# The first dense product placed ahead of the last row's attention values, and three copies of constants moved from the third to the last group of the first expert

## The chip, the cores and the metric

One Trainium2 chip, one of its cores. The metric is the device time of one execution in microseconds (us). Engines are named as the profile names them: PE is TensorE (PEld is its weight load), DVE is VectorE, ACT is ScalarE, POOL is GpSimd, SP is SyncE, which here only issues DMAs (SPq is its queue).

## What is computed

The program runs three layers after each other, all in float32 (here cut to what matters):

```python
# attention, B=2 H=8 S=768 D=64: only keys in the query's hash bucket count
scores = np.where(q_bucket[..., :, None] == k_bucket[..., None, :], scale * q @ k.T, -1e9)
x = softmax(scores) @ v                      # -> [1536, 512]
# first mixture, dense: every expert computes every token
P = sinkhorn(x @ w_gate)                     # 8 rounds of row and column sums
x = sum(P[:, e:e+1] * (relu(x @ w1[e]) @ w2[e]) for e in range(8))
# second mixture, routed: each token goes to one expert, or to none
out = x;  out[chosen] += gate * (relu(x @ w1[e_idx]) @ w2[e_idx])
```

## The kernel before

Each engine has its own program, and they meet at semaphores. The core's work comes in three stages: attention up to about 249 us, the dense mixture (8 experts of about 106 us) up to about 1157 us, then the routed one.

**Attention.** There are 96 row tiles of 128 queries (16 heads of 6). For each, PE computes the scores, turns the probabilities (`turn`, L1596) and multiplies them by the values (`values`, 18 small matmuls on L1606, L1608 and L1610). ACT evicts the turned probabilities as a rounded float16 part, and DVE takes the rest as a second part, `probsT_lo` (L1096). `values` of a tile waits for that. The last tile's `values` stands alone behind the loop over pairs of heads. DVE then scales its result (`normalise_last`, up to L1127), which lets PE turn the second batch's x (`turn_x`, L1641).

**An expert of the dense mixture.** The first matrix product is a fast scheme of 7 products instead of 8. `expert` on PE runs 8 groups (g = 0 to 7). A group is seven calls of `group_product`, six matmuls of 128x384 each (L1699, L1701, L1702). The first four write four PSUM banks, and the other three add into them. Each product needs the parts of one block of x (`x7_hi` and `x7_lo`), which POOL, ACT and DVE make from `xf`: POOL sums and splits on L687 to L705, ACT rounds on L852, DVE takes the remainder on L1153. In the first expert `x_parts` waits for them. DVE combines the banks (L1254, L1262 to L1269) and splits the result for the second product (L1258, L1351). ACT copies one bank (L927, `x1s`). Then PE runs 12 row tiles (t = 0 to 11) of the second product, 24 matmuls of 128x512 each (L1673, L1676, L1677), alternating between two banks, so tile t waits until DVE has emptied tile t - 2.

**What the first expert does besides.** The 8 rounds of the gate are woven into its 12 row tiles. Behind tile t DVE copies the tile out (L1306) and does one round of the gate (L1225 to L1243), ending in `columns_in`. Behind tile t PE waits for `columns_in` to reach t, and sums over the partitions with a small matmul (L1795). At t = 1, 2, 4, 5, 7, 8 and 10 DVE also makes the low part of a block of the next expert's first weights (`w1_part`, L1197), for which ACT must have made the high part (L896) from `wf`. ACT waits for all four loads of `wf`. POOL sums blocks of it (L625 to L636), each behind one more round of the gate.

**SP's queue.** SP issues its DMAs in the order of its program. After the second weights of expert 0 it stands as follows: SP first waits for three signs of `blank_ready`, two of which come from DVE's copies in the diff. `rows` is the buffer in HBM in which the routed stage collects tokens. The loop then brings the next expert's weights into `wf`, whose buffer is free once DVE has made the last part of w2 (behind group 6).

```python
sp.wait_ge(blank_ready, 3)
sp.dma_start(row_tiles, blank[...].to_broadcast(...)).then_inc(blanked, 16)   # L462
with sp.Fori(1, E) as e:
    sp.wait_ge(w2_lo_ready, DT * e)
    load_w1(w1_of[bass.ds(e, 1)]...)          # L442, four DMAs of 512 KB into wf
```

Of the kernel before, what the change touches and what calls it, by code (L numbers as in the profile page):

```python
# [26 lines left out]
G = B * H  # L27
QT = S // P
NTILES = G * QT
# [69 lines left out]
def build(nc, qT, kT, v, proj, consts, gates, w1a, w2a, w1b, w2b, rows, out):  # L99
    ctx = ExitStack()  # L100
    with ctx:
# [250 lines left out]
        def group_bank(g, role):  # L352

            return ps[:, (4 * g + role) % 6, 0:HT]
# [717 lines left out]
        def _(dve):  # L1072
# [173 lines left out]
            def expert(e, first, last):  # L1246
                for g in range(NGROUPS):
                    b, i = divmod(g, FH)
                    products_done, groups_done = e * NM1 + NP * g, e * NGROUPS + g
                    now, before = parts[g % 2], parts[(g - 1) % 2]  # L1250

                    dve.wait_ge(p1_copied, groups_done + 1)
                    dve.wait_ge(mm1_done, products_done + 2)
                    dve.tensor_tensor(now[:, 0, :], group_bank(g, 1), x1s[:, :], ALU.add).then_inc(u2_ready, 1)  # L1254
                    if g > 0:
                        split_rest(g - 1, groups_done - 1, before)
                    dve.wait_ge(hi11_ready, groups_done + 1)
                    dve.scalar_tensor_tensor(out=h[:, b, 1, i, 0, :], in0=group_bank(g, 0), scalar=0.0,  # L1258
                                             in1=h[:, b, 0, i, 0, :], op0=ALU.max, op1=ALU.subtract
                                             ).then_inc(lo11_ready, 1)  # L1260
                    dve.wait_ge(mm1_done, products_done + 6)
                    dve.tensor_tensor(now[:, 1, :], group_bank(g, 1), x1s[:, :], ALU.add).then_inc(u3_ready, 1)  # L1262
                    dve.wait_ge(u3_ready, groups_done + 1)
                    dve.wait_ge(p5_copied, groups_done + 1)
                    dve.tensor_tensor(now[:, 2, :], now[:, 2, :], now[:, 1, :], ALU.add).then_inc(c22_ready, 1)
                    dve.tensor_tensor(now[:, 1, :], group_bank(g, 3), now[:, 1, :], ALU.add).then_inc(c21_ready, 1)
                    dve.wait_ge(u2_ready, groups_done + 1)
                    dve.wait_ge(mm1_done, products_done + 7)
                    dve.tensor_tensor(now[:, 0, :], group_bank(g, 2), now[:, 0, :], ALU.add).then_inc(c12_ready, 1)  # L1269
                    if first and g == 4:  # L1270
                        split_gates()
                    if first and g == 2:
                        dve.tensor_copy(earlier16[:, :], const[:, C_EARLIER:C_EARLIER + P]).then_inc(setup_ready, 1)
                        dve.wait_ge(xt_turned, TT)
                        dve.tensor_copy(x[:, :, DM + 1:DM + 2].bitcast(uint32), const[:, C_TOKEN:C_TOKEN + TT].unsqueeze(2)
                                        ).then_inc(blank_ready, 1)
                        dve.tensor_copy(blank[:, DM + 1:DM + 2].bitcast(uint32), const[:, C_NONE:C_NONE + 1]
                                        ).then_inc(blank_ready, 1)
                    if first and g in (2, 3):
                        for k in X_SUMS[2 * (g - 2):2 * (g - 1)]:  # L1280
                            x7_lo_part(1, k)
                    for c in W2_FIRST.get(g, ()) if first else (g,) if g < 4 else ():
                        w2_part(e, c)
                    if first and g == 6:
                        dve.wait_ge(logits_done, 1)
                        add_logit_parts()
                        dve.tensor_reduce(top1[:, :], logits[:, :, :], AX.XY, ALU.max
                                          ).then_inc(top_ready, 1)
                    if first and g == 7:
                        dve.wait_ge(top_ready, 2)  # L1290
                        dve.tensor_scalar(top_bias[:, :], top_all[:, :], -1.0 / (X_SCALE * W_SCALE), None,
                                          ALU.mult).then_inc(top_ready, 1)
# [54 lines left out]
            def split_rest(g, groups_done, now):  # L1347

                b, i = divmod(g, FH)
                dve.wait_ge(hi3_ready, groups_done + 1)  # L1350
                dve.scalar_tensor_tensor(out=h[:, b, 1, i, 1:4, :], in0=now[:, :, :], scalar=0.0,  # L1351
                                         in1=h[:, b, 0, i, 1:4, :], op0=ALU.max, op1=ALU.subtract
                                         ).then_inc(lo3_ready, 1)
# [207 lines left out]
        def _(pe):  # L1561
# [37 lines left out]
            def values(i, g, q, r, head_r):  # L1599
                pe.wait_ge(probsT_lo_ready, 2 * i + 2)  # L1600
                if q == 0:
                    pe.wait_ge(v_split, 3 * g + 3)
                    reached(pe, o_taken, g)
                for k in range(QT):
                    keys = slice(k * P, (k + 1) * P)
                    pe.matmul(psO[:, q, :], probsT_hi[r][:, keys], V_hi[head_r][:, k, :],  # L1606
                              start=(k == 0), stop=False)
                    pe.matmul(psO[:, q, :], probsT_hi[r][:, keys], V_lo[head_r][:, k, :],  # L1608
                              start=False, stop=False)
                    last = pe.matmul(psO[:, q, :], probsT_lo[r][:, keys], V_hi[head_r][:, k, :],  # L1610
                                     start=False, stop=(k == QT - 1))
                last.then_inc(pv_done, 1)
# [50 lines left out]

            head_pairs(pe, pair)

            values(NTILES - 1, G - 1, QT - 1, 1, 1)

            def products(acc, pairs, before=lambda m: None, begun=None):

                n = len(pairs)  # L1670
# [35 lines left out]
            def expert(e, first, last_one):  # L1706
                pe.wait_ge(w1_lo_ready, NP * e + NP)
                for g in range(NGROUPS):
                    b, i = divmod(g, FH)
                    groups_done = e * NGROUPS + g  # L1710

                    def x_parts(k):
                        if first and i == 0:
                            pe.wait_ge(*((x7_lo_dve, len(X_SUMS) * b + X_SUMS.index(k) + 1) if k in X_SUMS else
                                         (x7_lo_pool, len(X_BLOCKS) * b + X_BLOCKS.index(k) + 1)))

                    def bank_free(role):

                        n = 4 * g + role - 6
                        if n >= 0:  # L1720
                            freed = (lo11_ready, u3_ready, c12_ready, c21_ready)[n % 4]
                            pe.wait_ge(freed, e * NGROUPS + n // 4 + 1)

                    bank_free(0)
                    x_parts(0)
                    group_product(g, 0, 0, 0, True)
                    bank_free(1)
                    x_parts(1)
                    group_product(g, 1, 4, 1, True)
                    bank_free(2)  # L1730
                    x_parts(2)
                    group_product(g, 2, 3, 2, True)
                    if first and g == 1:
                        turn_x(QT + 4)
                        turn_x(QT + 5)
                    bank_free(3)
                    x_parts(3)
                    group_product(g, 3, 2, 3, True)
                    pe.wait_ge(p1_copied, groups_done + 1)
                    x_parts(4)  # L1740
                    group_product(g, 0, 1, 4, False)
                    if first and g == 0:
                        turn_x(QT)
                        turn_x(QT + 1)
                    pe.wait_ge(u2_ready, groups_done + 1)
                    x_parts(5)
                    group_product(g, 1, 5, 5, False)
                    pe.wait_ge(p5_copied, groups_done + 1)
                    x_parts(6)
                    group_product(g, 2, 6, 6, False)  # L1750
                    if first and g == 0:
                        turn_x(QT + 2)
                        turn_x(QT + 3)
                    if first and g == 5:
                        pe.wait_ge(gates_split, 2)
                        pe.wait_ge(xf_ready, TT)
                        for t in range(TT):
                            last = logit_columns(ps[:, 7, t * 2 * E:(t + 1) * 2 * E], t, gates16[0])
                        last.then_inc(logits_done, 1)
# [72 lines left out]
            def rank_tokens(group):  # L1832
# [27 lines left out]
                last.then_inc(rank_done, 1)  # L1860

            experts(pe, expert)


# [173 lines left out]
```

## Time and profile before

| | |
|---|---|
| median of 3 runs | 1353.08 us (1351.26 to 1353.22) |
| profiled execution, its own time | 1349.94 us |
| span of its profile | 1348.1 us |
| PE busy | 1313.8 us, 97% of the span |
| DVE busy | 844.6 us, 63% |
| ACT busy | 566.4 us, 42% |
| POOL busy | 291.4 us, 22% |
| moved by DMA | 109.84 MB, mean 81 GB/s |

All times of single instructions below are counted from the start of the span. An idle time in brackets behind an instruction says how long its engine sat idle before it, and what released it. PE's matmuls are pipelined, so their durations overlap: the distance from one start to the next is what a matmul costs.

### The profile page before, as it was taken

The page shows a single profiled execution, that of the slowest core. Times are in us where ns is not written, and L with a number is a line of the kernel's source. Part 1 is how long each engine was busy: PE and PEld are TensorE (multiplying, and loading weights), DVE is VectorE, ACT ScalarE, POOL GpSimd, SP SyncE. Part 2 cuts the span into 40 slices and gives each one's busy share as a digit, 9 for nine tenths or more (in the row PEclk, how much of TensorE's full clock was granted, in tenths as well). Part 3 has the DMA queues.
Part 4 walks back from the last instruction along what each step waited for, and adds up shares of the span by engine and source line. Part 5 has one row for each costly group of instructions (what it writes and reads, how often), then busy time and mean ns, then how long its engine had stood idle before and what let it go on. Part 6 is the DMA issues. An engine that isn't in the chain of part 4 may idle for free.

```text
span 1348.1 us, 24739 instructions
## 1 busy us (share of the span) xinstructions
PE 1313.8 (97%) x9435; PEld 760.2 (56%) x9435; DVE 844.6 (63%) x1487; ACT 566.4 (42%) x868; POOL 291.4 (22%) x251
## 2 busy tenths in 40 slices
PE   6999999999999999999999999999999999999987
PEld 3776667655455456445545644654564465556665
DVE  5999999686576247436634742762464375568983
ACT  5999999642134114304312420440242043226662
POOL 3667666623002000300300030030003000121211
PEclk9999999999999999999999999999999999999999
DMA  9344441051011011001101100100110122468940
GB/s 239 94 115 110 107 114 52 20 205 63 1 63 63 1 63 62 0 0 65 59 0 62 62 0 17 72 36 0 62 62 0 43 79 82 155 216 296 343 154 21
DMA packets 51632, 109.84 MB, mean 81 GB/s; under 512 B 5216, under 2 KB 8840, under 8 KB 51568
## 3 DMA queue, kind: packets, MB, share of 16 engines
q1 hardware_dynamic: 48880, 105.40, 24.8%
q0 software_dynamic: 2240, 3.35, 0.7%
q8 instruction: 45, 0.74, 0.2%
q10 hardware_dynamic: 448, 0.19, 0.1%
q14 instruction: 19, 0.16, 0.0%
HBM read 93.57 MB, written 17.34 MB: 82 GB/s over the span
## 4 chain that ended last, share of the span: by engine, by line
PE 92%; DVE 3%; ACT 2%; issue 1%; DMA 1%; SPq 1%; POOL 0%; ACTq 0%; POOLq 0%; DVEq 0%
PE ps L1673 14%; PE ps L1676 14%; PE ps L1677 14%; PE ps L1699 11%; PE ps L1702 11%; PE ps L1701 11%; PE ps L1596 5%; PE ps L1584 2%; PE ps L1586 2%; PE ps L1568 2%; PE ps L1606 1%; PE ps L1608 1%; PE ps L1610 1%; ACT probsT_hi L811 1%; DMA qk_in<-kT 1%
## 5 line engine op out<-in xcount | busy, mean ns | idle before, releaser
L1699 PE MATMUL ps<-x_hi,w_hi 128*128 128x384 f16 x896 | 292.1, 326 | 1.9 <-DVE parts L1254 1.1
L1702 PE MATMUL ps<-x_hi,w_lo 128*128 128x384 f16 x896 | 292.1, 326 | 0.0
L1701 PE MATMUL ps<-x_lo,w_hi 128*128 128x384 f16 x896 | 292.1, 326 | 0.0
L1677 PE MATMUL ps<-w_hi,h 128*128 128x512 f16 x768 | 291.0, 379 | 0.0
L1676 PE MATMUL ps<-w_lo,h 128*128 128x512 f16 x768 | 291.0, 379 | 0.0
L1673 PE MATMUL ps<-w_hi,h 128*128 128x512 f16 x768 | 291.0, 379 | 0.0
L1311 DVE SCALAR_TENSOR_TENSOR x<-ps,gate_now,x 128x512 f32<-128x512 f32 x84 | 63.1, 751 | 251.7 <-PE ps L1677 250.8
L927 ACT ACTIVATE x1s<-ps 128x384 f32<-128x384 f32 x64 | 30.4, 475 | 327.3 <-PE ps L1702 327.3
L625 POOL TENSOR_TENSOR wf<-wf 128x1024 f32<-128x1024 f32 x8 | 18.8, 2354 | 633.4 <-PE ps L1702 622.5
L944 ACT ACTIVATE h<-parts 128x1152 f16<-128x1152 f32 x64 | 74.4, 1163 | 141.4 <-DVE parts L1269 141.4
L1677 PEld LDWEIGHTS ps<-w_hi,h 128*128 128x128 f16 x768 | 75.1, 98 | 90.6
L1673 PEld LDWEIGHTS ps<-w_hi,h 128*128 128x128 f16 x768 | 75.8, 99 | 86.3
L1676 PEld LDWEIGHTS ps<-w_lo,h 128*128 128x128 f16 x768 | 75.1, 98 | 86.3
L1699 PEld LDWEIGHTS ps<-x_hi,w_hi 128*128 128x128 f16 x896 | 87.7, 98 | 60.5 <-DVE parts L1254 1.5
L1702 PEld LDWEIGHTS ps<-x_hi,w_lo 128*128 128x128 f16 x896 | 87.7, 98 | 57.9
L1701 PEld LDWEIGHTS ps<-x_lo,w_hi 128*128 128x128 f16 x896 | 87.7, 98 | 57.9
L1096 DVE TENSOR_TENSOR probsT_lo<-ps,probsT_hi 128x384 f16<-128x384 f32 x192 | 97.8, 550 | 11.7 <-ACT probsT_hi L811 10.1
L804 ACT ACTIVATE probs<-ps,row_bias,row_scale 128x768 f32<-128x768 f32 x96 | 95.3, 993 | 0.8
L1351 DVE SCALAR_TENSOR_TENSOR h<-parts,h 128x1152 f16<-128x1152 f32 x64 | 87.7, 1371 | 10.4 <-ACT h L944 10.4
L1102 DVE TENSOR_REDUCE row_max<-ps 128x1 f32<-128x768 f32 x96 | 91.0, 948 | 4.2 <-PE ps L1586 4.2
L1596 PE MATMUL ps<-const,probs 128*128 128x128 f32 x576 | 85.9, 283 | 2.6 <-DVE probsT_lo L1096 1.8
L811 ACT ACTIVATE probsT_hi<-ps 128x384 f16<-128x384 f32 x192 | 83.4, 490 | 8.2 <-PE ps L1596 7.3
(228 smaller groups left out, 2235.7 us busy)
## 6 DMA issues: line engine op xcount, KB each, us to landing
wf<-w1a SPq DMA_DIRECT2D x32, 512.0 KB, 6.0
w_stage_in<-w2a SPq DMA_DIRECT2D x8, 2048.0 KB, 8.9
w_in<-w1b SPq DMA_DIRECT2D x4, 2048.0 KB, 9.6
w_in<-w2b SPq DMA_DIRECT2D x4, 2048.0 KB, 9.6
w_in_b<-w1b SPq DMA_DIRECT2D x4, 2048.0 KB, 10.2
w_in_b<-w2b SPq DMA_DIRECT2D x4, 2048.0 KB, 10.0
rows<-blank SPq DMA_DIRECT2D x1, 6682.0 KB, 21.5
qk_in<-kT SPq DMA_DIRECT2D x32, 192.0 KB, 4.5
```

The costliest lines, as they stand in the source:

```text
L804: act.activation(probs[r][:, :], psS[r], ACT.Exp, bias=row_bias[:, slot:slot + 1], scale=row_scale[:, slot:slot + 1]).then_inc(probs_ready, 1)
L811: act.activation(probsT_hi[r][:, half * HALF:(half + 1) * HALF], psT[half], ACT.Copy).then_inc(probsT_hi_ready, 1)
L1096: dve.tensor_tensor(probsT_lo[r][:, keys], psT[half], probsT_hi[r][:, keys], ALU.subtract).then_inc(probsT_lo_ready, 1)
L1102: dve.tensor_reduce(row_max[:, slot:slot + 1], psS[r], AX.X, ALU.max).then_inc(max_ready, 1)
L1351: dve.scalar_tensor_tensor(out=h[:, b, 1, i, 1:4, :], in0=now[:, :, :], scalar=0.0, in1=h[:, b, 0, i, 1:4, :], op0=ALU.max, op1=ALU.subtra ...
L1596: last = pe.transpose(psT[half][:, k * P:(k + 1) * P], probs[r][:, keys], ident)
L1673: first = pe.matmul(acc, a_hi, b_hi, start=(m == 0), stop=False)
L1676: pe.matmul(acc, a_hi, b_lo, start=False, stop=False)
L1677: last = pe.matmul(acc, a_lo, b_hi, start=False, stop=(m == n - 1))
L1699: pe.matmul(group_bank(g, role), w_hi, x_hi, start=(opens and kt == 0), stop=False, skip_group_check=not opens)
L1701: pe.matmul(group_bank(g, role), w_hi, x_lo, start=False, stop=False, skip_group_check=not opens)
L1702: last = pe.matmul(group_bank(g, role), w_lo, x_hi, start=False, stop=(kt == 1), skip_group_check=not opens)
```

## The change

The last tile's `values` moves behind the first product of expert 0's first group. DVE's three copies of constants, which stood behind group 2, now stand behind group 7. The copies make `earlier16` (a triangle of ones in bfloat16 for the ranks of the routed stage), the column of token numbers in `x`, and the last column of `blank`.

```diff
@@ DVE, expert(), in the loop over groups g
-                    if first and g == 2:
+                    if first and g == 7:
                         dve.tensor_copy(earlier16[:, :], const[:, C_EARLIER:C_EARLIER + P]).then_inc(setup_ready, 1)
                         dve.wait_ge(xt_turned, TT)
                         dve.tensor_copy(x[:, :, DM + 1:DM + 2].bitcast(uint32), const[:, C_TOKEN:C_TOKEN + TT].unsqueeze(2)
                                         ).then_inc(blank_ready, 1)
                         dve.tensor_copy(blank[:, DM + 1:DM + 2].bitcast(uint32), const[:, C_NONE:C_NONE + 1]
                                         ).then_inc(blank_ready, 1)
@@ PE, behind the attention loop
             head_pairs(pe, pair)
 
-            values(NTILES - 1, G - 1, QT - 1, 1, 1)
-
@@ PE, expert(), in the loop over groups g
                     bank_free(0)
                     x_parts(0)
                     group_product(g, 0, 0, 0, True)
+                    if first and g == 0:
+                        values(NTILES - 1, G - 1, QT - 1, 1, 1)
                     bank_free(1)
                     x_parts(1)
                     group_product(g, 1, 4, 1, True)
```

PE at the end of attention, before. The first two rows are the end of the `values` of tile 94, the others the first of the 18 matmuls of tile 95 (the last one):

```order
L1608 MATMUL ps<-V_lo1,probsT_hi0 128x65
L1610 MATMUL ps<-V_hi1,probsT_lo0 128x65
L1606 MATMUL ps<-V_hi1,probsT_hi1 128x65
L1608 MATMUL ps<-V_lo1,probsT_hi1 128x65
L1610 MATMUL ps<-V_hi1,probsT_lo1 128x65
L1606 MATMUL ps<-V_hi1,probsT_hi1 128x65
```

The same place of the changed kernel (its dense matmuls stand two lines higher in the file):

```order
L1608 MATMUL ps<-V_lo1,probsT_hi0 128x65
L1610 MATMUL ps<-V_hi1,probsT_lo0 128x65
L1697 MATMUL ps<-x7_hi,w7_hi 128x384
L1699 MATMUL ps<-x7_lo,w7_hi 128x384
L1700 MATMUL ps<-x7_hi,w7_lo 128x384
L1697 MATMUL ps<-x7_hi,w7_hi 128x384
L1699 MATMUL ps<-x7_lo,w7_hi 128x384
L1700 MATMUL ps<-x7_hi,w7_lo 128x384
L1606 MATMUL ps<-V_hi1,probsT_hi1 128x65
```

The six matmuls of product 0 now stand between the values of tile 94 and those of tile 95.

DVE, both places of the copies, as the difference of before and after (`x_lo` is the remainder of the second batch's x, `h` and `parts` belong to the group):

```order
 L1269 TENSOR_TENSOR parts<-ps,parts 128x384
-L1273 CAST earlier<-const 128x128
-L1275 CAST x<-const 128x12
-L1277 CAST blank<-const 128x1
 L1153 TENSOR_TENSOR x_lo<-x_sums,x_hi 128x768 x2
 L1254 TENSOR_TENSOR parts<-ps,x1s 128x384
@@ -292,4 +289,7 @@
 L1266 TENSOR_TENSOR parts<-ps,parts 128x384
 L1269 TENSOR_TENSOR parts<-ps,parts 128x384
+L1273 CAST earlier<-const 128x128
+L1275 CAST x<-const 128x12
+L1277 CAST blank<-const 128x1
```

The two `x_lo` of group 2 follow the group's last combination directly now, and the copies stand behind the last combination of group 7.

SP's queue around the large DMA. It reads the same in both kernels, with the semaphores it waits for:

```order
L460 DMA w_stage_in<-w2a 128x8x512 [waits w1_lo_ready]
L462 DMA rows<-blank 128x26x514 [waits blank_ready]
L465 UNCONDITIONAL_BRANCH
L465 ISA
L442 ISA [waits w2_lo_ready]
L442 DMA wf<-w1a 128x2x512
```

Nothing moves here, but the sign for which L462 waits is given five groups later.

## Rows read from the trace of the kernel before

**Rows 1.** The page, part 1: busy time and share of each engine.

```profile
PE 1313.8 (97%) x9435; PEld 760.2 (56%) x9435; DVE 844.6 (63%) x1487; ACT 566.4 (42%) x868; POOL 291.4 (22%) x251
```

**Rows 2.** Timeline of PE: start us, us, instruction, idle time before it.

```profile
248.87 0.20 PE L1606 MATMUL ps<-V_hi,probsT_hi 128*128 128x65 f16 x1 [0.74 <-DVE probsT_lo L1096]
...
249.44 0.33 PE L1699 MATMUL ps<-x_hi,w_hi 128*128 128x384 f16 x1
...
254.31 1.04 PE L1641 MATMUL ps<-const,x_attn 128*128 128x128 f32 x8
...
279.66 0.34 PE L1699 MATMUL ps<-x_hi,w_hi 128*128 128x384 f16 x1 [1.10 <-DVE parts L1254]
```

**Rows 3.** Timeline of POOL, columns as in rows 2.

```profile
237.20 1.65 POOL L705 TENSOR_TENSOR x_lo<-xf,x_hi 128x768 f16<-128x768 f32 x1
...
269.08 1.64 POOL L705 TENSOR_TENSOR x_lo<-xf,x_hi 128x768 f16<-128x768 f32 x1
...
275.54 1.64 POOL L705 TENSOR_TENSOR x_lo<-xf,x_hi 128x768 f16<-128x768 f32 x1
...
319.78 2.33 POOL L625 TENSOR_TENSOR wf<-wf 128x1024 f32<-128x1024 f32 x1 [10.97 <-DVE column_sum L1243]
```

**Rows 4.** Timeline of DVE up to group 3, columns as in rows 2.

```profile
248.73 3.55 DVE L1153 TENSOR_TENSOR x_lo<-x_sums,x_hi 128x768 f16<-128x768 f32 x4
...
252.62 0.56 DVE L1127 TENSOR_TENSOR x_attn<-ps,denom 128x384 f32<-128x384 f32 x1
...
269.19 2.75 DVE L1351 SCALAR_TENSOR_TENSOR h<-parts,h 128x1152 f16<-128x1152 f32 x1
...
275.62 1.65 DVE L1273 CAST earlier<-const 128x128 bf16<-128x128 f32 x1
...
277.32 1.81 DVE L1153 TENSOR_TENSOR x_lo<-x_sums,x_hi 128x768 f16<-128x768 f32 x2
...
279.52 1.34 DVE L1351 SCALAR_TENSOR_TENSOR h<-parts,h 128x1152 f16<-128x1152 f32 x1
```

**Rows 5.** Timeline of SP's queue: issue of DMAs.

```profile
277.43 0.40 SPq L462 DMA_DIRECT2D rows<-blank  x1
```

**Rows 6.** The page, part 6: KB, and us from issue to landing.

```profile
rows<-blank SPq DMA_DIRECT2D x1, 6682.0 KB, 21.5
```

**Rows 7.** Landing of the four loads of `wf` issued 307.7 to 309.4.

```profile
DMA to landing us min/median/max: 3.7/5.3/6.9
```

**Rows 8.** Busy time by stretch: PE, PEld, DVE, ACT, POOL, clock, DMA share, GB/s.

```profile
296.00:300.00 4.00, 4.00 (x108) 3.35 (x105) 2.85 (x4) 1.65 (x2) 0.00 (x0) 1.00 0.26 85
307.00:317.00 10.00, 10.00 (x56) 5.29 (x54) 6.88 (x13) 4.08 (x7) 0.38 (x1) 1.00 0.60 211
```

**Rows 9.** Timeline of ACT: the next expert's first weights.

```profile
316.40 2.95 ACT L896 ACTIVATE w_hi<-wf 128x1024 f16<-128x1024 f32 x3 [1.61 <-DMA wf<-w1a]
```

**Rows 10.** Timeline of DVE, group 7 and row tile 1.

```profile
312.69 0.55 DVE L1269 TENSOR_TENSOR parts<-ps,parts 128x384 f32<-128x384 f32 x1
...
322.48 0.69 DVE L1306 COPY x<-ps 128x512 f32<-128x512 f32 x1 [3.20 <-PE ps L1677]
...
323.52 0.26 DVE L1228 TENSOR_TENSOR Pm<-Pm,column_sum 128x96 f32<-128x96 f32 x1
...
325.10 1.22 DVE L1197 SCALAR_TENSOR_TENSOR w_lo<-wf,w_hi 128x1024 f16<-128x1024 f32 x1
```

**Rows 11.** Timeline of PE: its partition sum behind row tile 3.

```profile
332.91 0.28 PE L1795 MATMUL ps<-column_sum,ones 128*128 128x8 f32 x2
```

**Rows 12.** Timeline of PE near the program's start, attention scores.

```profile
12.72 0.61 PE L1584 MATMUL ps<-K,Q 76*128 76x512 f16 x1 [3.79 <-DVE A L1146]
...
14.40 0.63 PE L1586 MATMUL ps<-A 128*128 128x512 f16 x1
...
21.99 0.38 PE L1586 MATMUL ps<-A 128*128 128x512 f16 x1
```

**Rows 13.** Busy time of the last stretch, columns as in rows 8.

```profile
1341.00:1348.00 7.00, 0.00 (x0) 0.00 (x0) 0.72 (x1) 0.00 (x0) 0.97 (x1) 0.83 0.07 25
```

## The prediction

> **What bounds the kernel now.** I read the page first. PE is busy for 97% of the span [rows 1], so time is won where PE idles and lost where PE is made to idle. Then I listed PE's idle times between 240 and 333 us. Two of them matter here: 0.74 us ahead of the last tile's `values`, released by DVE's `probsT_lo`, and 1.10 us in group 3, released by DVE's L1254 [rows 2]. Last I followed the consumers of the three copies. None sits near the copies on DVE. Two of them release SP's DMA of `blank`, issued at 277.43 just as the copies end [rows 4, 5]. It carries 6682 KB and lands 21.5 us after issue [rows 6]. SP issues it ahead of the next expert's weights, which were issued from 307.7 to 309.4 [rows 7]. Today the large DMA is finished by then: in 296 to 300 us the DMA engines are busy for 0.26 of 4 us, so its traffic ends near 297.0 [rows 8].
>
> All clock times below are those of before. The changed kernel will be earlier by what the front edit wins.
>
> **Edit 1, product 0 ahead of `values`.** The last `values` start at 248.87 after 0.74 us of idleness; the matmul in front lasts 0.19 and the 18 are about 0.03 apart, so PE could have gone on at 248.87 - 0.74 - 0.19 + 0.03 = 247.97. The 18 take until 249.44, or 0.57 us. Between 249.44 and 254.31 lie five products, 0.97 us each [rows 2]. Product 0's operands are there: POOL wrote its `x_lo` at 237.20, for 1.65 us [rows 3]. So product 0 runs from 247.97 to 248.94 and the values to 249.51. Product 1 would then start 0.90 us earlier than before, when it started at 249.44 + 0.97 = 250.41. It needs the first of DVE's four `x_lo`, though. They start at 248.73, take 3.55 us together [rows 4], and so about 0.95 for the first. That ends at 249.68, and with the signal it is 249.74. The gain is **0.67 us**, 0.90 at most. The values now end 0.07 us later. Their consumer is DVE's `normalise_last`, which stands behind the four `x_lo` (ended at 252.28) and is not delayed; it ends at 252.62 + 0.56 = 253.18 [rows 4], ahead of PE's `turn_x`, now at 254.31 - 0.66 = 253.65. So the transposes are not late either, and the chain from there (transposes, ACT's `xf`, POOL's sums) moves up with PE.
>
> **Edit 2, the copies leave group 2.** The three lie between the last combination and two `x_lo`, from 275.62 to 277.40. `earlier` alone takes 1.65 us, and it began 0.08 us after POOL's 1.64 us L705 and ended 0.09 after it (275.54 + 1.64 = 277.18) [rows 3, 4]. DVE's L1351 shows the same: 2.75 us where it began beside POOL's L705 at 269.08, 1.34 in group 3 [rows 3, 4]. So what stood there was a wait for POOL, and I expect `x_lo`, which also reads two operands of the on-chip buffer, to inherit it. Then the first `x_lo` starts to stream at 277.18 and ends near 277.99, the second at 278.87, against 277.32 + 1.81 = 279.13. That wins 0.26 us of PE's 1.10. If DVE got in ahead of POOL, all 1.10 would be won. I take **0.26**, since a common shift moves both engines together and POOL began first by 0.08.
>
> **The copies arrive in group 7.** DVE's L1269 there ends at 313.24 [rows 10]. POOL works on nothing then. `earlier` costs between the 0.14 of a tiny DVE instruction and its own 1.65; I take 0.25, since the other bound was a wait for POOL. From the end of `earlier` to the issue of the DMA it was 277.43 - 277.27 = 0.16 [rows 4, 5]. So the DMA of `blank` is issued at about 313.16 + 0.25 + 0.16 = **313.6** instead of 277.4. On DVE itself the copies hide in the wait for ACT in front of the last L1351.
>
> **What is queued behind it.** The next expert's four weight DMAs were ready to go at 307.7. SP issues in program order, so they leave after 314. They also lie behind 6682 KB in the same queue. The large DMA's traffic ended 297.0 - 277.4 = 19.6 us after its issue, so it now ends at 333.2. The four need 0.60 x 10 = 6.0 us of the DMA engines [rows 8], to 339.2. Do DMAs of one queue go one after the other? The four of `wf` landed 3.7 us (least) to 6.9 us (most) after issues that were 1.7 us apart [rows 7]. If they had shared the engines evenly, the first would have landed near the last; instead it was there at 307.7 + 3.7 = 311.4 and the last at 309.4 + 6.9 = 316.3. That is one after the other. ACT began on the weights at 316.40 [rows 9], about 1.1 us after the traffic's end (309.3 + 6.0 = 315.3), so now at **340.3** instead of 316.4.
>
> The Trainium skill (DMA: Bandwidth & Descriptors, Queues, rings and completion order) says that the engines take turns between queue rows only, and that within one row's ring descriptors are consumed in order. The landings just told agree. It also says that completion isn't first in, first out across engines. If that let the weights through early, the time would be that of the first rival below.
>
> **Who waits.** ACT's first high part takes about 1.04 us (three in 2.95, overlapping slightly [rows 9]): 341.35. DVE's L1197 for it stands behind row tile 1, where DVE arrives at 325.10 [rows 10]. DVE then sits there, and behind it in its queue are the copy of row tile 2, the gate's third round and `columns_in`. PE finishes row tiles 2 and 3 and comes to the sum at 332.91 [rows 11], which needs just that round. From there PE idles. POOL starts on the weights at 340.3 too, 2.33 us on L625 [rows 3], so L1197 meets it as L1351 did: it ends at 342.63 + 1.08 = 343.7. From the copy's start to the next L1197 it is 325.10 - 322.48 = 2.62 us [rows 10], and POOL's next sum (2.3 us, from 343.7 to 346.0) can hold up L1228, which would start 1.04 us behind the copy [rows 10], by 1.3 us more. So `columns_in` comes at 343.7 + 2.62 + 1.3 + 0.1 = 347.7, and PE stalls for 347.7 - 332.9 = **14.8 us**. Without any wait for POOL: 341.35 + 1.2 + 2.7 = 345.3, or 12.4 us. With the first alone, 13.5. I take 14.8, because both meetings have the shape of the two that cost 1.4 and 1.5 us above.
>
> The Trainium skill (SBUF — State Buffer, SBUF: two separate sides) speaks against this change: POOL and a DVE instruction with two SBUF inputs exclude each other for a whole instruction, and whoever starts first holds. Rows 4 agree, with 2.75 against 1.34 us. By the page the stall is 14.8 us; for it to be 12.4 the page would have to be wrong here.
>
> **The clock.** PE's granted clock is 1.00 in the stretches of rows 8. In the last 7 us, with PE idle, its mean is 0.83 [rows 13], so it fell to the lower level (1.2 GHz) within them, and it will fall in a gap of 14.8 us. Matmuls at the lower level show near the start: 0.63 us for 128x512 at 14.40, after a pause of 3.79 us, against 0.38 for the same shape at 21.99 [rows 12]. Resuming slow costs at least 0 and at most half of the 21.99 - 12.72 = 9.3 us in which the clock came back, 4.6 us. I take **2.0**, since that stretch had pauses of its own. Tile 4 being slow gives DVE and POOL time to catch up, so no further stall follows; at most 1 us.
>
> **The sum.** 1349.94 - 0.67 - 0.26 + 14.8 + 2.0 = 1365.8 us for a profiled execution. The median of the runs shown is 3.1 us above the profiled one, so 1353.1 + 15.9 = **1369.0 us**.
>
> **Rivals.**
> 1. *The two transfers share the DMA engines, or the weights pass.* Then the weights land by 315 + 2 x 6 + 1 = 328 at the latest, DVE's L1197 ends by 331, the third round by 334, and PE waits 1 us at most (up to 3.6 with waits for POOL). Time 1352.2 with no wait, up to 1355. The issue order allows it; the landings of the four speak against it. If they land by about 329 this rival decides. This is the case on the other side, not slower. Chance 0.07.
> 2. *The stall is shorter than its waits for POOL, and the clock is harmless*: +12.4 - 0.9 = 11.5, so 1364.6. It is inside the forecast's mechanism: chance 0.2. The skill's lock and the rows 12 and 13 speak against it.
> 3. *The large DMA is slow beside other traffic, or tile 4 stalls again*: +14.8 + 4.6 + 1 - 0.9 = 19.5, so 1372.6. Chance 0.15.
> 4. *The copies' move does nothing, and both idle times of PE close*: 0.90 + 1.10 = 2.0 us, so 1351.1. It would take the weights to land as early as now, against the queue's order. Chance 0.03.
>
> The forecast itself has 0.55. Its range is 1366 to 1371. Taking in rivals 2 and 3, and 1.5 us for the runs' own scatter (1351.26 to 1353.22), 1362.5 to 1373 should hold 8 in 10. A measurement of this kernel can tell about 0.2% (2.7 us) from no change. Slower than that: 0.55 + 0.2 + 0.15, and 0.01 of rival 1, is 0.91. Within it: 0.06 of rival 1 and 0.01 of rival 4, 0.07. Faster: 0.02 of rival 4.
>
> **What would show it.** In the changed kernel's profile: no idle time of PE between tile 94's values and product 0; the first two `x_lo` of the second batch taking about 3.2 us instead of 1.81 and starting right behind L1269; SP issuing L462 near 312.7 and the four loads right behind; the high parts of `wf` on ACT starting near 339.4 with a wait for the DMA; one idle time of PE of 12 to 15 us ahead of L1795 with DVE's column sum as releaser; then some slow matmuls of 0.6 us. The prediction is wrong if the weights land before 329, or if DVE finds its first high part in time.

## The result

| | before | changed kernel |
|---|---|---|
| median | 1352.17 us (1349.28 to 1353.22, 4 runs) | 1367.79 us (1364.87 to 1371.05, 4 runs) |
| profiled execution, its own time | 1349.94 us | 1371.05 us |
| span of its profile | 1348.1 us | 1369.2 us |

The changed kernel is slower: 1.0122 of before, 95% interval 1.0104 to 1.014, or 14 to 19 us. 1369.0 was forecast, with a range of 1366 to 1371.

The page of the changed kernel, parts 1 and 6. PE and DVE are busy for 6.4 and 3.6 us longer than in [rows 1], and the span is 21.1 us longer. So most of what came on top is idle time of PE.

```profile
PE 1320.2 (96%) x9435; PEld 764.4 (56%) x9435; DVE 848.2 (62%) x1487; ACT 566.4 (41%) x868; POOL 291.3 (21%) x251
...
rows<-blank SPq DMA_DIRECT2D x1, 6682.0 KB, 21.7
```

PE's waits of the changed kernel between 230 and 420 us (engine, line, releaser; then us in all, how many, the longest). One wait outweighs all others, and its releaser is the gate's column sum on DVE. The 0.74 us ahead of the last values [rows 2] isn't among them any more.

```profile
PE ps L1795 <- DVE column_sum L1243: 14.9, 1, 14.9
PE ps L1596 <- DVE probsT_lo L1096: 1.3, 2, 0.8
PE ps L1697 <- DVE parts L1254: 0.8, 1, 0.8
PE ps L1697 <- ACT x1s L927: 0.8, 1, 0.8
```

To read this wait back to its cause, one goes from engine to engine. SP's queue first: the large DMA leaves at 312.75 instead of 277.43 [rows 5]. The issue of the four weight loads begins right behind it, and alone keeps SP for 15.58 us (2.06 before).

```profile
312.75 0.40 SPq L462 DMA_DIRECT2D rows<-blank  x1
313.91 15.58 SPq L442 DMA_DIRECT2D wf<-w1a  x4
```

Of these four, the issues (least, median and most ns; start of the first and the last) and the landings (us, least, median and most):

```profile
L442 SPq DMA_DIRECT2D wf<-w1a x4: 1182/1465/10912, 313.9 to 327.7; - x4
...
DMA to landing us min/median/max: 12.0/12.0/21.7
```

If the last one took the least time, it landed at 327.7 + 12.0 = 339.7. ACT, which waits for all four, starts 0.2 us later, POOL with it. Both timelines:

```profile
339.92 2.95 ACT L896 ACTIVATE w_hi<-wf 128x1024 f16<-128x1024 f32 x3 [25.93 <-DMA wf<-w1a]
```

```profile
340.01 2.35 POOL L625 TENSOR_TENSOR wf<-wf 128x1024 f32<-128x1024 f32 x1 [31.99 <-DMA wf<-w1a]
342.32 3.31 POOL L628 TENSOR_TENSOR wf<-wf 128x1024 f32<-128x1024 f32 x1
```

DVE's timeline, from `w_lo` (L1197) to the column sum for which PE waits. L1197 waits 16.62 us for ACT's high part, and the gate's round stands behind it in the same queue.

```profile
341.01 2.43 DVE L1197 SCALAR_TENSOR_TENSOR w_lo<-wf,w_hi 128x1024 f16<-128x1024 f32 x1 [16.62 <-ACT w_hi L896]
343.36 0.68 DVE L1306 COPY x<-ps 128x512 f32<-128x512 f32 x1
...
344.38 1.37 DVE L1228 TENSOR_TENSOR Pm<-Pm,column_sum 128x96 f32<-128x96 f32 x1
...
346.84 0.32 DVE L1243 TENSOR_REDUCE column_sum<-Pm 128x8 f32<-128x96 f32 x1
```

PE's timeline: the turn of x, the wait, and row tile 4 behind it. The 128x512 matmuls take about 0.6 us up to 353 (the first 14 of the 24 of row tile 4), and the last column sum of these rows starts at 355.78. From one sum to the next it is 8.57 us, where before it was 338.23 - 332.91 = 5.32.

```profile
253.81 1.04 PE L1641 MATMUL ps<-const,x_attn 128*128 128x128 f32 x8
...
347.21 0.60 PE L1795 MATMUL ps<-column_sum,ones 128*128 128x8 f32 x2 [14.92 <-DVE column_sum L1243]
347.66 0.59 PE L1671 MATMUL ps<-w_hi,h 128*128 128x512 f16 x1
...
353.17 0.62 PE L1674 MATMUL ps<-w_lo,h 128*128 128x512 f16 x1
353.59 0.41 PE L1675 MATMUL ps<-w_hi,h 128*128 128x512 f16 x1
...
355.78 0.28 PE L1795 MATMUL ps<-column_sum,ones 128*128 128x8 f32 x2
```

The windows (columns of rows 8) give the granted clock in the sixth column of busy times: a mean of 0.88 over the first 6 us of PE's idleness, then 0.50, the lower of its two levels (1.2 of 2.4 GHz), up to 353, then 1.00. The last two rows belong to the routed stage, to which I come below.

```profile
332.00:338.00 6.00, 0.29 (x2) 0.00 (x0) 0.00 (x0) 0.00 (x0) 0.00 (x0) 0.88 1.02 354
340.00:347.00 7.00, 0.00 (x0) 0.00 (x0) 5.75 (x10) 2.87 (x3) 5.63 (x2) 0.50 0.00 0
348.00:350.00 2.00, 2.00 (x6) 0.76 (x5) 1.93 (x5) 0.00 (x0) 2.00 (x1) 0.50 0.00 0
353.00:354.00 1.00, 1.00 (x4) 0.38 (x3) 0.00 (x0) 0.00 (x0) 1.00 (x1) 0.68 0.00 0
354.00:356.00 2.00, 2.00 (x13) 1.09 (x11) 0.01 (x1) 1.45 (x2) 0.43 (x1) 1.00 0.00 0
...
1235.00:1240.00 5.00, 1.33 (x8) 0.71 (x7) 1.87 (x3) 1.88 (x4) 0.37 (x2) 0.77 0.86 273
1240.00:1245.00 5.00, 5.00 (x53) 5.00 (x52) 3.86 (x4) 1.01 (x3) 2.10 (x2) 0.55 0.99 373
```

At 1209 us 17.56 of the span's 21.1 us are in place, and nothing came on top in the seven experts between: SP's next load of w2 (L470) was already 17.55 us late (390.85 against 373.30). These experts take 116.8 us each, from one load of `wf` to the next (405.10 and 521.86 before), and not the 106 us given at the start. SP's DMA L513 is the landmark at 1209, first in the kernel before, then in the changed one.

```profile
1191.53 0.34 SPq L513 DMA_DIRECT2D xg<-rows  x1
```

```profile
1209.09 0.34 SPq L513 DMA_DIRECT2D xg<-rows  x1
```

### The profile page after: what moved, and what is told of

Its sections match the earlier page's. It is cut to its first block, busy times and chain, and to the rows that moved or that the text cites. A ratio compares the mean times of both kernels' runs of the same rounds, so it can differ in the third digit from the quotient of the medians.

```text
span 1369.2 us, 24739 instructions
## 1 busy us (share of the span) xinstructions
PE 1320.2 (96%) x9435; PEld 764.4 (56%) x9435; DVE 848.2 (62%) x1487; ACT 566.4 (41%) x868; POOL 291.3 (21%) x251
## 4 chain that ended last, share of the span: by engine, by line
PE 90%; DVE 4%; DMA 2%; SPq 2%; issue 1%; ACT 1%; POOL 0%; POOLq 0%; ACTq 0%; DVEq 0%
PE ps L1671 14%; PE ps L1674 14%; PE ps L1675 14%; PE ps L1697 11%; PE ps L1700 10%; PE ps L1699 10%; PE ps L1596 6%; PE ps L1584 2%; PE ps L1586 2%; PE ps L1568 2%; PE ps L1606 1%; PE ps L1608 1%; PE ps L1610 1%; SPq L442 1%; DMA wf<-w1a 1%
## 5 line engine op out<-in xcount | busy, mean ns | idle before, releaser
L625 POOL TENSOR_TENSOR wf<-wf 128x1024 f32<-128x1024 f32 x8 | 18.8, 2356 | 655.8 <-PE ps L1700 623.8
```

## The experiments

The time of before is that of the runs made with each experiment. "Changed" is the kernel with both edits.

**The front edit alone** (label e1).

```diff
-            values(NTILES - 1, G - 1, QT - 1, 1, 1)
...
                     group_product(g, 0, 0, 0, True)
+                    if first and g == 0:
+                        values(NTILES - 1, G - 1, QT - 1, 1, 1)
```

> Only the front edit: product 0 ahead of the last values, the copies stay behind group 2. My theory: PE's 0.74 us of idleness ahead of the values is gone, product 1 starts about 0.67 us earlier relative to DVE's first x_lo, group 3 still idles for about 0.8 and 1.1 us, and no long idle time appears: about 0.7 us less than before, a ratio near 0.9995, no difference that can be told. Rival (the front edit costs something in the stall, by delaying the normalisation): a transpose of the second batch's x waits, and the time is 1 to 3 us more.

Measured: 1351.12 us (12 runs) against 1352.75 (23 runs), ratio 0.999 (0.998 to 0.9999). The long wait is absent, no transpose of x waits, the copies of constants still meet POOL, and the weights leave at once. The interval of the ratio is 0.1 to 2.7 us; the 0.7 expected lies in it.

**The copies' move alone** (e2).

```diff
-                    if first and g == 2:
+                    if first and g == 7:
```

> Only the copies moved to group 7, the values where they were. Theory (SP's queue): the whole loss is here: PE idles for about 14.9 us ahead of its sum behind row tile 3, and its clock then costs about 3.2 us more, minus 0.3 us in group 3: about 17.9 us more than before, ratio near 1.013. Rival (the loss needs both edits): under 5 us more.

Measured: 1369.76 us, ratio 1.0136 (1.0117 to 1.0155), or 17.0 us more. PE's timeline has the whole stall, and the sum behind row tile 4:

```profile
346.47 0.59 PE L1795 MATMUL ps<-column_sum,ones 128*128 128x8 f32 x2 [15.37 <-DVE column_sum L1243]
...
353.99 0.28 PE L1795 MATMUL ps<-column_sum,ones 128*128 128x8 f32 x2
```

The loss belongs to this edit, and with the 1.6 us that e1 won it adds up to +15.4 us, against +15.6 for both edits together. Row tile 4 takes 353.99 - 346.47 = 7.52 us here, 1.05 less than in the changed kernel's profile, though PE's wait in front of it is longer.

**The weights ahead of the large DMA** (e3): the changed kernel, but SP issues the loads of expert 1 before it waits for `blank_ready`.

```diff
+            sp.wait_ge(w2_lo_ready, DT)
+            load_w1(w1_of[1])
             sp.wait_ge(blank_ready, 3)
             sp.dma_start(row_tiles, blank[...].to_broadcast(...)).then_inc(blanked, 16)
+            sp.wait_ge(w1_lo_ready, 2 * NP)
+            sp.dma_start(w2_stage_in[:, :, :], w2_of[1]).then_inc(w2_loaded, 16)
-            with sp.Fori(1, E) as e:
+            with sp.Fori(2, E) as e:
```

> The changed kernel with one thing different: SP issues the four loads of the next expert's first weights ahead of the large DMA of blank. The same bytes, the same copies at group 7. Theory (order in SP's queue): the stall is gone, and what is left is the gain of the front edit and of group 3: 0.9 to 1.0 us under before, ratio near 0.9993. Rival (the copies themselves or the large transfer's traffic at that time hold DVE, ACT or PE up): a good part of the 15 us stays.

Measured: 1352.21 us (12 runs), ratio 0.9996 (0.9986 to 1.0006); the 0.9 to 1.0 us of gain expected can't be told from nothing. SP's timeline has the loads at their old time and in 2.23 us, with the same large DMA behind them:

```profile
307.64 2.23 SPq L442 DMA_DIRECT2D wf<-w1a  x4
313.60 0.39 SPq L464 DMA_DIRECT2D rows<-blank  x1
```

Both edits and the late DMA are still there; only the order in the queue differs, and the loss is gone. The DMA's lateness costs nothing by itself.

**Half the large DMA ahead** (e4): the fill is cut into halves of 13 row tiles, and the weights stand between them (POOL waits for both halves).

```diff
             sp.wait_ge(blank_ready, 3)
-            sp.dma_start(row_tiles, blank[...].to_broadcast(...)).then_inc(blanked, 16)
+            sp.dma_start(row_tiles[:, 0:half, :], ...).then_inc(blanked, 16)
+            sp.wait_ge(w2_lo_ready, DT)
+            load_w1(w1_of[1])
+            sp.dma_start(row_tiles[:, half:, :], ...).then_inc(blanked, 16)
```

> The changed kernel with the large DMA in two halves: 13 of its 26 row tiles ahead of the four weight loads, 13 behind. Theory (one after the other): the weights land by half of the large transfer earlier, 9.3 us, so the first high part starts near 330.5 instead of 339.9 and PE idles for 5 to 6 us instead of 14.9; with some of the slow clock the time is 5 to 8 us over before. Rival (the two transfers share the DMA engines): they would then move 2 x 2 MB until the weights are there, 12 us from 313.9, by 327, and PE would idle for under 2 us.

Measured: 1360.32 us, ratio 1.0061 (1.0041 to 1.008). SP's, ACT's and PE's timelines: from the issue of the fill to ACT's start it is 330.60 - 311.52 = 19.08 us, against 339.92 - 312.75 = 27.17 in the changed kernel. So the weights come 8.1 us earlier, and PE waits 8.1 us less. (The plain difference of ACT's starts, 9.3 us, takes in 1.2 us by which this trace runs ahead from before the fill.)

```profile
311.52 0.41 SPq L463 DMA_DIRECT2D rows<-blank  x1
```

```profile
330.60 2.95 ACT L903 ACTIVATE w_hi<-wf 128x1024 f16<-128x1024 f32 x3 [17.83 <-DMA wf<-w1a]
```

```profile
337.89 0.59 PE L1802 MATMUL ps<-column_sum,ones 128*128 128x8 f32 x2 [6.83 <-DVE column_sum L1250]
```

Half the bytes ahead take away 8.1 us, where half of the 19.6 that the whole took is 9.8; PE waits 6.8 us, where 5 to 6 were expected. No run explains the missing 1.7 us. Had the two transfers shared the engines evenly, the weights would have been there by 327 here, and PE would have waited under 2 us. That did not happen.

**PE kept busy in the wait** (e5): the changed kernel with 65 matmuls of no use, into a free bank, ahead of the wait for round 3.

```diff
+                        if t == 3:
+                            pe.wait_ge(c12_ready, NGROUPS)
+                            for n in range(65):
+                                pe.matmul(ps[:, 2, :], w2_hi[:, 0, 0:P], w2_hi[:, 1, :], start=True, stop=True)
                         pe.wait_ge(columns_in, t)
```

> The changed kernel with 65 extra matmuls of 128x512 on PE (14.0 us at 0.216 us each), into a bank that nobody reads, in the place where PE waits for the gate's sum behind row tile 3. They compute nothing that is used. Theory (the slow clock is a cost of its own beside the wait): the gate's sum still comes at about the same time as in the changed kernel (347.2 us), but row tile 4 runs at full speed in about 5.2 us instead of 8.1, so the time is 3.2 us under the changed kernel's, about 12.3 us over before. Rival (the slow matmuls are due to something else, such as ACT's, POOL's and DVE's traffic on the weights): row tile 4 still takes about 8 us and the time is as in the changed kernel.

Measured: 1365.33 us, ratio 1.0096 (1.0081 to 1.0111). PE's timeline and the window over the wait:

```profile
332.59 14.19 PE L1797 MATMUL ps<-w_hi 128*128 128x512 f16 x65
348.21 0.39 PE L1799 MATMUL ps<-column_sum,ones 128*128 128x8 f32 x2 [1.43 <-DVE column_sum L1243]
...
353.63 0.28 PE L1799 MATMUL ps<-column_sum,ones 128*128 128x8 f32 x2
```

```profile
332.00:347.00 15.00, 14.78 (x69) 6.51 (x67) 4.92 (x6) 2.95 (x3) 5.66 (x2) 1.00 0.50 166
```

The clock stays at 1.00, and row tile 4 takes 353.63 - 348.21 = 5.42 us instead of 8.57. So resuming at the lower clock cost 3.15 us in the changed kernel's profile, and the wait itself is untouched: the sum comes 35.0 us after the issue of the fill (313.21 here), against 34.5. In the medians the difference is 13.2 against 15.6 us over before, and the intervals of the two ratios overlap, so the saving is read from the trace.

**POOL's sums one round later** (e6): the changed kernel, with POOL's first sums held back so that they don't meet DVE.

```diff
-            sum_w1(1, lambda n: pool.wait_ge(columns_in, n + 1))
+            sum_w1(1, lambda n: pool.wait_ge(columns_in, max(n + 1, 3)))
```

> The changed kernel with POOL's sums of the next expert's first weights held back until the gate's third round is in (they waited for the first and the second before). Theory (DVE's L1197 and L1228 each wait for a POOL instruction): L1197 takes 1.2 us instead of 2.4 and L1228 0.26 instead of 1.37, PE's wait is 12.6 us instead of 14.9, and nothing later waits: about 2.3 us under the changed kernel. Rival (those two are long for another reason): L1197 and L1228 keep their lengths and PE's wait stays at 14.9 us. Third: the sums then come too late for the block of row tile 5, and PE waits there instead.

Measured: 1368.62 us, ratio 1.0119 (1.0104 to 1.0134), not to be told from the changed kernel. DVE's and PE's timelines:

```profile
341.98 1.23 DVE L1197 SCALAR_TENSOR_TENSOR w_lo<-wf,w_hi 128x1024 f16<-128x1024 f32 x1 [17.23 <-ACT w_hi L896]
...
344.15 0.26 DVE L1228 TENSOR_TENSOR Pm<-Pm,column_sum 128x96 f32<-128x96 f32 x1
```

```profile
345.88 0.60 PE L1795 MATMUL ps<-column_sum,ones 128*128 128x8 f32 x2 [13.23 <-DVE column_sum L1243]
...
354.50 0.39 PE L1795 MATMUL ps<-column_sum,ones 128*128 128x8 f32 x2 [0.56 <-DVE column_sum L1243]
```

The meetings with POOL are gone: L1197 takes 1.23 instead of 2.43 us, L1228 0.26 instead of 1.37, together the 2.3 expected. But DVE began 0.6 us later against PE in this execution, so PE's wait shrank by only 1.7 (14.92 + 0.6 - 2.3 = 13.2), and 0.56 came back a tile later, where DVE met POOL's delayed sum. The size of the meetings is confirmed; that they are worth their sum in time is not.

**Only the copy of `earlier` late** (e7): the front edit, and the two copies that release the large DMA stay in group 2.

```diff
-                    if first and g == 2:
+                    if first and g == 7:
                         dve.tensor_copy(earlier16[:, :], ...)
+                    if first and g == 2:
                         dve.wait_ge(xt_turned, TT)
```

> Front edit as in the changed kernel, but of the three copies only the triangle for the ranks goes to group 7. The two copies that release the large DMA stay in group 2, and SP's order is untouched. Theory (only the signal's time matters): the large DMA is issued near 275.5, the weights land as before near 316, PE never waits behind row tile 3, and the time is that of e3, 0.5 to 1 us under before. Rival (the traffic beside group 3 costs something that the late copies had avoided): over e3 by more than 1 us.

Measured: 1351.46 us (10 runs) against 1351.46 (29 runs), ratio 0.9996 (0.9985 to 1.0007). The DMA leaves at 276.25, there is no stall, but no gain from the place left free either (PE still waits 1.0 us in group 3). DVE's timeline shows why:

```profile
274.58 1.59 DVE L1276 CAST x<-const 128x12 uint32<-128x12 f32 x1
```

The copy of 12 columns, 0.17 us long before, now stands where `earlier` stood, beside POOL's L705 (274.50, for 1.64 us), and takes over the wait for it.

**POOL behind DVE in group 2** (e8): e3, with POOL's last split of the second batch held back until DVE's two `x_lo` are done.

```diff
+                if b == 1 and k == 6:
+                    pool.wait_ge(x7_lo_dve, len(X_SUMS) + 2)
```

> The kernel with the weights ahead of the large DMA (e3), and POOL's last split of the second batch held back until DVE has made its first two x_lo of that batch. Theory (in group 3 the two x_lo wait for POOL's L705): they take 1.8 us instead of 3.2, PE's wait of 0.8 us ahead of L1254's product in group 3 is gone, and the time is up to 0.8 us under e3, too little to tell by the clock on the wall but to be read in the profile. Rival (a wait that moves): the held-back L705 then meets DVE's L1351 in group 3, and PE waits elsewhere for as long.

Measured: 1350.86 us (11 runs) against 1352.13 (23 runs), ratio 0.9987 (0.9978 to 0.9997). DVE's timeline: the two `x_lo` take 1.81 us again (3.24 in the changed kernel) and start at 274.04, ahead of POOL, which now takes 2.62 instead of 1.64 us.

```profile
274.04 1.81 DVE L1159 TENSOR_TENSOR x_lo<-x_sums,x_hi 128x768 f16<-128x768 f32 x2
```

PE's wait for L1254 is gone, and of the two waits in that group in e3 (0.82 us for ACT's `x1s`, 0.83 for L1254's successor in that file, L1258) only the first is left. The meeting that the rival named does take place (DVE's split of h takes 1.76 us instead of 1.34), but PE does not wait for it.

**PE kept busy in two pauses** (e9: e3 with 10 and 6 matmuls of no use around PE's wait for the second tile of gathered rows in the routed stage; e10: that and 36 and 32 short ones around the first hash products at the start). The edit of e9:

```diff
+            keep_busy(10)
             pe.wait_ge(rows_loaded[0], rows_loads(0))
...
             turn_row_tile(1, 0)
+            keep_busy(6)
             pe.wait_ge(r_xt_lo, CS)
```

> The kernel e3 with 16 extra matmuls of 128x512 whose result nobody reads, in the routed stage: 10 ahead of PE's wait for the rows of expert 0's second tile (2.3 us of idleness) and 6 behind the four transposes that follow (1.4 us). Theory (the runs of one kernel differ by whether PE's clock falls in that pause): the clock reads 1.00 from 1215 to 1240 us in the profile, and the median is 1 to 2 us under e3, with a smaller spread. Rival (the spread comes from elsewhere, for instance the start of the program): the median is as in e3 or the 16 matmuls cost up to 0.5 us.

> The kernel e9 with small extra matmuls (128x128, result unread) in PE's two pauses before its first scores: 36 ahead of the first hash product and 32 behind the two. Theory (the first scores, 0.63 us for 128x512, run at the lower clock because of the pauses ahead of them): they take 0.38 us, their starts lie 0.22 us apart, and the start of attention is 1 to 3 us earlier; the median is 1 to 2 us under e9. Rival (the first scores are slow whatever PE did before, or the start is bound by ACT and DVE): the median is as in e9.

Measured: e9 1351.21 us, ratio 0.9991 (0.9981 to 1.0001), with the clock at 1.00 from 1190 to 1240. By the ratio it can't be told from before, and the spread of its runs, expected smaller, is that of e3 (1349.1 to 1353.73 against 1348.96 to 1353.69). e10 1350.8 us, ratio 0.9992 (0.9981 to 1.0003), no gain over e9, where 1 to 2 us were expected: the first scores are fast, as PE's timeline shows, but the clock falls in the next pause:

```profile
12.39 0.39 PE L1588 MATMUL ps<-K,Q 76*128 76x512 f16 x1 [2.53 <-DVE A L1150]
...
17.71 0.58 PE L1588 MATMUL ps<-K,Q 76*128 76x512 f16 x1 [2.38 <-ACT probs L808]
```

**All that helped** (e11: both edits, the weights first, e8, e9 and e10).

> All that helped together: product 0 first, copies at group 7 with the weights ahead of the large DMA, POOL's last split behind DVE's two x_lo (e8), and the extra matmuls of e10 in the pauses. Theory: the gains add, 0.8 us of e8 on top of e10: 3 to 4 us under before, ratio 0.997 to 0.998, and a smaller spread of the runs. Rival: as e10 or e8 alone, within 1 us.

Measured: 1349.24 us (1348.56 to 1351.84, 12 runs) against 1351.46 (1348.34 to 1354.7, 29 runs), ratio 0.9983 (0.9974 to 0.9993). It has the lowest median of the study: 2.2 us under before, where 3 to 4 were expected, and its runs lie closer together. Which of its parts brought this is not shown.

## Why the prediction was right

**The front edit.** 0.67 us forecast. The turn of x starts at 253.81 instead of 254.31, while DVE's and POOL's clocks stand 0.16 us later in this trace throughout the end of attention, so the gain is 0.66. That it reaches the end is not shown: e1's interval of 0.1 to 2.7 us holds it, those of e3 and e7, which have this edit too, also hold no gain at all.

**The place left free in group 2.** 0.26 forecast, with `x_lo` inheriting the wait. DVE's timeline of the changed kernel:

```profile
275.10 3.24 DVE L1153 TENSOR_TENSOR x_lo<-x_sums,x_hi 128x768 f16<-128x768 f32 x2
278.27 0.55 DVE L1254 TENSOR_TENSOR parts<-ps,x1s 128x384 f32<-128x384 f32 x1
```

The two `x_lo` take 3.24 us (3.2 forecast), and PE's wait there went from 1.10 to 0.83: the product behind it starts at 278.87 instead of 279.66, which is 0.29 more than the 0.50 that the front edit had brought. e7 and e8 settle the cause: each of the three instructions that came to stand there waited (`earlier`, the copy of 12 columns, `x_lo`), and with POOL held back `x_lo` did not. The Trainium skill (SBUF — State Buffer, SBUF: two separate sides) has this as a mutual exclusion of POOL and two-input DVE instructions for a whole instruction. The 3.24 against 1.81 us agree. Under conditions on their operands it names copies and casts with one input as well, and the 1.59 us of e7's cast agree with that.

**The late signal and the queue.** The DMA was forecast for 312.7 in the changed kernel and left at 312.75; its copy took 0.21 us, 0.25 forecast. ACT was forecast for about 339.4 and began at 339.92. e3 shows that the queue's order alone makes the loss. The rival in which the transfers share the engines is out: it needed the weights by 329 here and by 327 in e4, and ACT began at 339.92 and 330.60. One thing came otherwise than forecast: the loads did not leave right behind the large DMA, since issuing them took 15.58 us and the last left at 327.7. No run separates this wait at the issue from the wait in the queue; ACT's start, which has both in it, came 0.5 us later than forecast.

**PE's wait.** 14.8 forecast, 14.92 measured, along the very chain forecast: L1197 in 2.43 us beside POOL's L625, then L1228 in 1.37 beside L628. e6 shows these two meetings as 2.3 us. The stall of 12.4 us of rival 2 is out with that, and so is the second stall of rival 3: the list of PE's waits has only one for L1795.

**The clock.** 2.0 forecast, 3.25 measured in the changed kernel's profile (8.57 - 5.32). There the term was too small. But the same stall does not have one price: in e2, after 15.37 us of idleness, it is 7.52 - 5.32 = 2.20. In both profiles the clock is back before row tile 4 ends; in the changed kernel's its first 14 matmuls run at the lower level, in e2's the first 9. So the bounds of 0 and 4.6 held, the 2.0 between them was a choice that no row gave, and which price the unprofiled runs paid is not known.

**The sum.** -0.66 - 0.29 + 14.92 + 3.25 = +17.2 us, against +15.9 forecast. The traces show +17.56 at 1209 us, 0.16 of it from ahead of the change. The medians differ by 15.6, and the interval of the ratio, 14 to 19 us, holds all of these. The remaining 1.8 us between traces and medians are not resolved; the clock term alone differs by 1.05 between two profiles, and single executions of one kernel differ by more (1349.8 to 1355.8 in the runs of before beside e1). That the medians differ by nearly the 15.9 forecast is therefore partly luck: the terms of the traces add up to 1.3 us more.

**The profiled execution** was, at 1371.05, the slowest of its four and 5.3 us over the 1365.8 forecast for it. 1.25 of that is the clock term. Another 2.9 us (20.46 - 17.56) came between the landmarks at 1209 and 1255 (SP's L489: 1234.38 before, 1254.84 now), where PE pauses for gathered rows and the clock then stands at 0.77 and 0.55, as the last two windows of the changed kernel show. In the profile of before, the clock stayed up in the same pause:

```profile
1217.00:1222.00 5.00, 1.71 (x15) 0.91 (x13) 2.52 (x5) 2.60 (x4) 0.37 (x2) 1.00 0.80 242
```

This isn't a price of the change. The kernel of e3, without any stall, shows the same fall there in its profile.

## What to carry to other kernels

A signal that nobody on the spot is waiting for may be the first condition of an in-order queue. Before moving it, list what stands behind the DMA it releases, not only who reads the data, and either move the DMA behind the urgent ones with it, or leave it. When an engine's idle time comes from another engine's hold, taking away the instruction that shows the wait only hands the wait to the next; hold the other engine back instead.

## What the runs showed of the hardware beyond that

- Issuing is itself held up behind a large transfer. Four loads took SP 15.58 us (one of them 10.91) behind 6682 KB, 15.72 in e2, 7.32 behind half of it (e4), and 2.06 to 2.23 with nothing ahead (before, e3). A signal or a load for someone else that stands next in that queue would be late too. Here nothing else stood there.
- A pause of 2.25 us and one of 1.41, with four short transposes between, let the clock fall in the changed kernel's profile, while 1.87 and 1.42 in the kernel before did not. It stayed up with a first pause of 1.91 us in e5 too, and fell with 1.97 in e6 and with 2.19 to 2.88 in e1 to e4, e7 and e8. This may be a part of the scatter of the runs: of the 23 runs of before beside e1, those with a mean clock of 0.998 took 1349.8 to 1350.3 us, the others (0.989 to 0.997) 1350.6 to 1355.8. In the two later sets of before the runs at 0.998 are among the short ones too (1348.5 to 1350.6), but the others reach as low (1348.3). Filling that pause goes with about 1 us in the median (e9 1351.21, e3 1352.21, from different sets of runs, so not shown).
- The clock column can hide a fall at the start. In the trace of before it reads 1.00 there, though the matmuls take 0.63 us [rows 12]; in e3's profile it reads 0.57, 0.50 and 0.65 between 12 and 24 us, with the same durations.
